# Fused tap mixing and two feed-forward layers: low parts made in other places and other forms

## What is computed

```python
def _attn_ref(x, weight):                       # x (2, 4096, 192), weight (8, 7)
    w = softmax(weight, axis=-1)
    x_pad = np.concatenate([zeros(B, 6, D), x], axis=1)
    x_unf = x_pad[:, idx, :].reshape(B, S, K, H, group)      # idx = s + k
    return np.einsum('hk,bskhg->bshg', w, x_unf).reshape(B, S, D)

def _moe_ref(x, w_gate, w_val, w_out):          # (8192, 192) -> 1536 -> 192
    g = x @ w_gate
    return (g * (1.0 / (1.0 + np.exp(-g))) * (x @ w_val)) @ w_out

def _moe2_ref(x, w_in, w_out):                  # (8192, 192) -> 2048 -> 192
    h = x @ w_in
    g = np.where(h > 0.0, h, np.exp(np.minimum(h, 0.0)) - 1.0)
    return g @ w_out
```

## Time and profile before

| | us |
|---|---|
| median of 3 runs | 1207.09 (1205.83 to 1207.34) |
| the profiled execution | 1206.76 |
| its span, first to last instruction | 1205.0 |
| PE busy (matmul) | 1199.5, 100% of the span |
| DVE busy | 775.5, 64% |
| POOL busy | 717.9, 60% |
| ACT busy | 664.2, 55% |
| granted TensorE clock | 1.000 in the whole span |

### The profile page before, as it was taken

The page is one execution under the profiler, slowest core; times in us unless marked ns, Lnnn a source line. Parts: engine busy times, 40 slices in busy tenths (PEclk is TensorE's granted clock), DMA queues, the critical chain, the costliest instruction groups (busy, mean ns, idle before and its releaser), DMA issues.

```text
span 1205.0 us, 31390 instructions
## 1 busy us (share of the span) xinstructions
PE 1199.5 (100%) x11798; PEld 1032.4 (86%) x11798; DVE 775.5 (64%) x1178; ACT 664.2 (55%) x1114; POOL 717.9 (60%) x528
## 2 busy tenths in 40 slices
PE   9999999999999999999999999999999999999999
PEld 7988888888888888889888898888988889888898
DVE  6787575675656756567665666656666476675665
ACT  6456555465554645546455464655546556465565
POOL 6787656574654746547465474654746557465565
PEclk9999999999999999999999999999999999999999
DMA  7412012120111211012110121100212002120110
GB/s 179 109 51 44 12 27 41 32 44 11 32 31 30 44 30 23 21 30 44 30 27 17 30 44 30 35 17 22 44 30 41 11 22 44 30 44 9 30 34 15
DMA packets 103955, 43.37 MB, mean 36 GB/s; under 512 B 75888, under 2 KB 93936, under 8 KB 103920
## 3 DMA queue, kind: packets, MB, share of 16 engines
q1 hardware_dynamic: 103104, 42.29, 15.7%
q10 hardware_dynamic: 816, 0.59, 0.2%
HBM read 16.12 MB, written 6.29 MB: 19 GB/s over the span
## 4 chain that ended last, share of the span: by engine, by line
PE 97%; POOL 1%; DVE 1%; issue 1%; ACT 0%; ACTq 0%; DVEq 0%
PE up L860 55%; PE down L860 42%; POOL hid_lo L441 1%; DVE mixed L830 0%; DVE act L771 0%; PE down L1063 0%; POOL up_w_lo L326 0%; DVE hidden L787 0%; ACT L617 0%; ACT hid_hi L608 0%; POOL y_main L445 0%; POOL halves L445 0%; DVE mixed L827 0%; DVE taps_head L813 0%; ACT act L593 0%
## 5 line engine op out<-in xcount | busy, mean ns | idle before, releaser
L441 POOL TENSOR_TENSOR hid_lo<-hidden,hid_hi 128x512 fp32r<-128x512 f32 x447 | 623.7, 1405 | 473.2 <-ACT hid_hi L574 304.8
L860 PE MATMUL down<-out_w,hid_hi 64*128 64x384 f32 x2040 | 300.4, 355 | 0.0
L734 DVE TENSOR_TENSOR hidden<-act,up 128x512 f32<-128x512 f32 x191 | 130.8, 685 | 249.1 <-ACT act L557 249.1
L860 PE MATMUL down<-out_w,hid_lo 64*128 64x192 f32 x2040 | 260.8, 251 | 0.3 <-POOL hid_lo L441 0.3
L771 DVE TENSOR_SCALAR act<-up 128x512 f32<-128x512 f32 x256 | 164.8, 685 | 112.0 <-PE up L860 112.0
L860 PE MATMUL up<-in_b_hi,up_w_hi 64*128 64x512 f32 x1128 | 224.1, 393 | 0.0
L860 PE MATMUL up<-in_b_hi,up_w_lo 64*128 64x512 f32 x1128 | 223.7, 393 | 0.0
L860 PE MATMUL up<-in_b_lo,up_w_hi 64*128 64x512 f32 x1128 | 223.6, 393 | 0.0
L574 ACT ACTIVATE hid_hi<-hidden 128x512 fp32r<-128x512 f32 x192 | 121.5, 633 | 177.9 <-DVE hidden L734 160.5
L608 ACT ACTIVATE hid_hi<-hidden 128x512 fp32r<-128x512 f32 x256 | 156.9, 628 | 96.5 <-DVE hidden L787 79.4
L593 ACT ACTIVATE act<-act 128x512 f32<-128x512 f32 x256 | 156.1, 631 | 94.8 <-DVE act L771 94.8
(11 more groups left out here) (96 smaller groups left out, 1085.9 us busy)
## 6 DMA issues: line engine op xcount, KB each, us to landing
x_raw<-x_dram SPq DMA_DIRECT2D x136, 64.0 KB, 2.2
out_dram<-stage SPq DMA_DIRECT2D x15, 384.0 KB, 2.7
in_b_hi<-in_b_hi SPq DMA_DIRECT2D x32, 128.0 KB, 2.3
in_b_lo<-in_b_lo SPq DMA_DIRECT2D x32, 128.0 KB, 2.3
swapped<-halves SPq DMA_DIRECT2D x32, 128.0 KB, 2.3
in_a_hi<-in_a_hi SPq DMA_DIRECT2D x30, 128.0 KB, 2.3
in_a_lo<-in_a_lo SPq DMA_DIRECT2D x30, 128.0 KB, 2.3
stage<-w_out_dram SPq DMA_DIRECT2D x7, 384.0 KB, 3.9
```

The source lines that it names most:

```text
L441: return pool.tensor_tensor(hid_lo[:, slot, :], hidden[:, s, :], hid_hi[:, slot, :].bitcast(F32), ALU.subtract)
L734: v.tensor_tensor(hidden[:, f % 2, :], act[:, f % 2, :], val_bank(f, n)[:, :], ALU.mult)\
L860: return nc.tensor.matmul(dst, lhsT, rhs, start=start, stop=stop, skip_group_check=True)
```

## The change

- `zero`, a tile of one column, is added, set by a further memset at the start (ZEROED 6 in place of 5).
- The first taps (steps 1 and 2 of `mix`) and `input_lo` become scalar-tensor-tensor instructions: x times tap plus `zero` (broadcast over 512 columns), and full times 1.0 less the high part.
- Chunk 1's taps, mixed beside chunk 0, follow a table `MIX_AT0`: 2, 3, 2, 2, 1, 3, 2, 1 steps behind products 2 to 9, and the two transposes stand behind product 2 in place of product 1. For all later chunks `MIX_AT` gives the old order.
- Piece 5 of the weights is split behind block 2 of chunk 0 in place of block 1, on ACT and POOL.
- The low part of piece 16 goes from DVE to POOL, at the same j; one semaphore `piece_lo` counts all low parts.

```diff
-        ZEROED = 5
+        ZEROED = 6
+        MIX_AT0 = {2: range(0, 2), 3: range(2, 5), 4: range(5, 7), 5: range(7, 9), 6: range(9, 10),
+                   7: range(10, 13), 8: range(13, 15), 9: range(15, 16)}
+        MIX_AT = {2: range(0, 1), **{3 + k: range(2 * k + 1, 2 * k + 3) for k in range(TAPS)},
+                  3 + TAPS: range(MIX - 1, MIX)}
...
-                              ("out", 1, "pool"), ("up", 6, "pool"), ("out", 2, "dve"), ("out", 3, "pool")):
+                         ("out", 1), ("up", 6), ("out", 2), ("out", 3)):
...
-        BESIDE0 = {1: 5, 3: 6, 5: 7, 7: 8, 8: 9}
+        BESIDE0 = {2: 5, 3: 6, 5: 7, 7: 8, 8: 9}
...
             eng.wait_ge(piece_hi, upto)
-            for who, made in (("dve", piece_lo_dve), ("pool", piece_lo_pool)):
-                if lo_count(upto, who):
-                    eng.wait_ge(made, lo_count(upto, who))
+            eng.wait_ge(piece_lo, lo_count(upto))
...
-                        v.tensor_scalar(mixed[:, part, :], src, tap, None, ALU.mult)\
-                            .then_inc(mix_step, 1)
+                        v.scalar_tensor_tensor(mixed[:, part, :], src, tap, zero[:, 0:1].broadcast_to([P, T]),
+                                               ALU.mult, ALU.add).then_inc(mix_step, 1)
...
-                v.tensor_tensor(dst["lo"][:, slot, :], full, dst["hi"][:, slot, :].bitcast(F32), ALU.subtract)\
-                    .then_inc(lo_sem, 1)
+                v.scalar_tensor_tensor(dst["lo"][:, slot, :], full, 1.0, dst["hi"][:, slot, :].bitcast(F32),
+                                       ALU.mult, ALU.subtract).then_inc(lo_sem, 1)
...
-                    if f == 1 and is_int(n, 0):
+                    if f == 2 and is_int(n, 0):
                         transpose_x(1, 0)
                         transpose_x(1, 1)
...
-                    at = 2 if is_int(n, 0) else 3
-                    if f == at - 1:
-                        mix(n + 1, 0)
-                    if at <= f < at + TAPS:
-                        mix(n + 1, 2 * (f - at) + 1)
-                        mix(n + 1, 2 * (f - at) + 2)
-                    if f == at + TAPS:
-                        mix(n + 1, MIX - 1)
+                    for step in (MIX_AT0 if is_int(n, 0) else MIX_AT).get(f, ()):
+                        mix(n + 1, step)
...
-            elu_phase(1, beside(BESIDE_ELU1, lambda i: make_lo(v, i, "dve")))
+            elu_phase(1)
```

More of the change, by code:

```diff
@@ L123, in mix_ffn_ffn @@
         y_tail = sb("y_tail", [P, T])
+        zero = sb("zero", [P, 1])
         result = stage[:, 0, :].rearrange("p (b d) -> p b d", d=D)
@@ L249, in up1_piece, with up2_piece @@
             hi, lo = up1_w["hi"][:, :, c0:c1], up1_w["lo"][:, :, c0:c1]
-            pieces.append((loads, [(hi, s)], [(lo, s, hi)], who))
-        def up2_piece(j0, j1, who):
+            pieces.append((loads, [(hi, s)], [(lo, s, hi)]))
+        def up2_piece(j0, j1):
             s = stage[:, len(pieces) % STAGES, 0:PARTS * (j1 - j0) * P].rearrange("p (g c) -> p g c", g=PARTS)
@@ L256, in up2_piece, with out_piece @@
             hi, lo = up2_w["hi"][:, :, j0 * P:j1 * P], up2_w["lo"][:, :, j0 * P:j1 * P]
-            pieces.append((loads, [(hi, s)], [(lo, s, hi)], who))
-        def out_piece(rows, dst, q, order, who):
+            pieces.append((loads, [(hi, s)], [(lo, s, hi)]))
+        def out_piece(rows, dst, q, order):
             s = stage[:, len(pieces) % STAGES, 0:OT * D].rearrange("p (f d) -> p f d", d=D)
@@ L263, in out_piece @@
             los = [(t[:, :, to:to + n], s[:, :, of:of + n], t[:, :, of:of + n]) for to, of, n in order]
-            pieces.append((loads, [(t[:, :, 0:D], s)], los, who))
+            pieces.append((loads, [(t[:, :, 0:D], s)], los))
         def out1_piece(q):
-            out_piece(wo1_rows, out1_w, q, [(D, P, TAIL), (D + TAIL, 0, P)], "pool")
+            out_piece(wo1_rows, out1_w, q, [(D, P, TAIL), (D + TAIL, 0, P)])
         UP1_AT, OUT1_AT = {}, {}
-        for what, at, who in (("up", 0, "pool"), ("up", 1, "pool"), ("up", 2, "pool"), ("out", 0, "pool"),
-                              ("up", 3, "pool"), ("up", 4, "pool"), ("out", 1, "pool"), ("up", 5, "pool"),
-                              ("up", 6, "pool"), ("out", 2, "pool")):
+        for what, at in (("up", 0), ("up", 1), ("up", 2), ("out", 0),
+                         ("up", 3), ("up", 4), ("out", 1), ("up", 5), ("up", 6), ("out", 2)):
             if what == "up":
-                up1_piece(at, who)
+                up1_piece(at)
                 UP1_AT[GROUPS[at][0] // P] = len(pieces)
@@ L281, in mix_ffn_ffn @@
         UP2_AT, OUT2_AT = {}, {}
[L282 to L283 removed]
+        for what, at in (("up", 0), ("up", 2), ("out", 0), ("up", 4),
+                         ("out", 1), ("up", 6), ("out", 2), ("out", 3)):
             if what == "up":
[L285 removed]
+                up2_piece(at, at + 2)
                 UP2_AT[at] = len(pieces)
             else:
[L288 removed]
+                out_piece(wo2_rows, out2_w, at, [(D, 0, D)])
                 OUT2_AT[at * OT] = len(pieces)
         AHEAD, READY = 6, 5
[L292 removed]
+        BESIDE0 = {2: 5, 3: 6, 5: 7, 7: 8, 8: 9}
         BESIDE1 = {0: 10, 1: 11, 9: 12, 10: 13, 11: 14}
@@ L299, in beside, with lo_count @@
             return lambda at: make(table[at]) if at in table else None
-        def lo_count(upto, who):
-            return sum(len(p[2]) for p in pieces[:upto] if p[3] == who)
+        def lo_count(upto):
+            return sum(len(p[2]) for p in pieces[:upto])
         def wait_weights(eng, upto):
             eng.wait_ge(piece_hi, upto)
-            for who, made in (("dve", piece_lo_dve), ("pool", piece_lo_pool)):
-                if lo_count(upto, who):
-                    eng.wait_ge(made, lo_count(upto, who))
+            eng.wait_ge(piece_lo, lo_count(upto))
         def stage_full(i):
@@ L319, in make_hi, with make_lo @@
                 nc.scalar.activation(dst, src, ACT.Copy).then_inc(piece_hi, 1)
-        def make_lo(eng, i, who):
-            if pieces[i][3] != who:
-                return
-            eng.wait_ge(piece_hi, i + 1)
+        def make_lo(pool, i):
+            pool.wait_ge(piece_hi, i + 1)
             for dst, src, hi in pieces[i][2]:
-                ins = eng.tensor_tensor(dst, src, hi.bitcast(F32), ALU.subtract)
-                ins.then_inc(piece_lo_dve if who == "dve" else piece_lo_pool, 1)
+                pool.tensor_tensor(dst, src, hi.bitcast(F32), ALU.subtract).then_inc(piece_lo, 1)
         def store_tokens(eng, m, blocks=slice(0, BLOCKS)):
@@ L490, in _ @@
             for i in range(READY):
[L491 to L492 removed]
+                make_lo(pool, i)
+            lo = lambda i: make_lo(pool, i)
             mix_phase(0, beside(BESIDE0, lo))
@@ L797, in _ @@
             v.memset(tap_pairs[:, :], 0.0).then_inc(zeroed, 1)
+            v.memset(zero[:, :], 0.0).then_inc(zeroed, 1)
             step = [0]
```

10 lines of the change are left out of this document (2 added, 8 removed).

## The result

The changed kernel takes **1208.96 us** in the median of 11 runs (1207.32 to 1209.72), the kernel before, run beside it, 1206.17 (11 runs, 1204.62 to 1207.46): a ratio of 1.002, interval 1.001 to 1.0029. It is slower by some 2.8 us, where the forecast was 0.8. The profiled execution took 1207.44, its span 1205.2, only 0.2 more than the span before. From that matmul on, the changed kernel is 1.4 us longer.

What follows compares the result with a forecast made beforehand. PE was taken as the bound, with no matmul removed. Chunk 0's +0.54 and piece 16's +0.28 gave +0.8 on the profiled 1206.76, 1207.6; the median's 0.33 above that execution made 1207.9, range 1206.0 to 1209.6.

Steps and rivals of the forecast that it cites:

- (c): Rival: the scalar-tensor-tensor form takes twice a tap's 0.74 us; +2.3 in chunk 0, 1209.4 in all; chance 0.05.
- (d): Rival: in chunk 0 one stall runs into the next, five blocks late by 0.3 to 0.5; +2, 1210; chance 0.09.
- `down1(0)` no longer waits: Block 3 of chunk 0: product 2 ends at 21.8, so PE's wait for it goes; minus 0.19 us.
- block 5: Chunk 0: product 3 comes just in time at 26.8 but PE finds its weights late; plus 0.08 us.
- block 6: Chunk 0: three taps ahead of product 4 delay PE's start from 30.21 to 30.48; plus 0.27 and 0.08 us.
- block 7: Chunk 0: product 5 was to end at 33.3, in time by 0.2 to 0.4; no loss for PE.
- block 10: Chunk 0: three taps ahead of product 8 take turns with POOL, product 8 at 43.75; plus 0.22 and 0.08 us.
- old losses of chunk 1: Second layer: both losses, 0.68 and 0.49, put down to piece 16 on DVE, would go; minus 1.17 us.
- wait for piece 16: Chunk 1's second layer: PE waits for POOL's piece 16 ahead of `down2_pair` of k = 8; plus 1.45, bounds 0.9 and 2.0.
- by the same steps product 5 ends at 33.3: Chunk 0: DVE and POOL taking turns as for product 4 would finish product 5 in time by 0.2 to 0.4 us.
- at a hand-over the one that has waited goes next: Timing rule for DVE's two-SBUF-input instructions against POOL's subtractions: whoever comes second ends 1.15 (POOL) or 0.55 (DVE) after the other.
- three signs of being wrong: A PE wait in the loop, piece 16 ending before 116, or taps with `zero` over 0.9 alone.

## Why the prediction was right in kind and too small

**The sum.** Forecast 1207.9 in a range of 1206.0 to 1209.6, measured 1208.96. The direction and the range are right, but the forecast of +0.8 is 2.0 short of the medians' difference. That the time still came within 1.1 is partly luck: the forecast started from a median of 3 runs, 1207.09, and the 11 beside the changed kernel gave 1206.17. The chances gave 0.90 to a difference under 2.4 us and 0.07 to a larger loss; the measured 2.8 is above that line, though its interval of 1.2 to 3.5 spans it. The upper part of the range was there for (c) and (d), which did not happen. Step by step, in what PE lost:

| term | forecast | traces of the changed kernel |
|---|---|---|
| `down1(0)` no longer waits | -0.19 | -0.26, with 0.07 at the pair behind |
| block 5 | +0.08 | +0.29 |
| block 6 | +0.35 | +0.29 |
| block 7 | 0 | +0.90 |
| block 10 | +0.30 | +0.44 |
| old losses of chunk 1 | -1.17 | -1.29, but in part of before's executions only |
| wait for piece 16 | +1.45 | +1.04; 1.48 or 1.49 in three relatives, where DVE gets in |

The last two rows are lengths of the second layer over the loop's 32.80; the forecast had missed 0.11 of the old losses, at the pair behind 122.32. The first five sum to +1.66, where the forecast had +0.54 and a bound of +1.5.

**The step that failed in chunk 0** is "by the same steps product 5 ends at 33.3", in time by 0.2 to 0.4. In the time scale of before (1.28 later) product 5 ended at 34.6. The rule beneath it, "at a hand-over the one that has waited goes next", does not hold for a tap issued 0.1 us ahead of the end of POOL's instruction, and piece 6 is two instructions in a row, so that missing one hand-over costs a whole further one. I had a lost hand-over in my bounds at half a microsecond. Here it cost the tap 1.24 (it ends at 31.04, and would have ended 0.55 behind POOL's 29.25), far more than my margin of 0.2 to 0.4. Moving piece 6 away removed exactly this loss. It is no draw: in all five traces with this order and piece 6 in its place, the tap is issued 0.08 ahead of the end and passed over. The trace of before had the same miss in a place I did not read, its first tap behind product 2:

```profile
22.25 3.60 DVE L686 TENSOR_SCALAR mixed<-x_t,taps 128x512 f32<-128x512 f32 x2
22.29 1.84 POOL L326 TENSOR_TENSOR up_w_lo<-stage,up_w_hi 128x768 fp32r<-128x768 f32 x1
```

POOL's instruction ahead of piece 5 ends at 22.33, 0.08 behind the tap's issue, and the tap still stands behind the whole piece and ends at 24.41.

**The step that failed in the second layer** is the same rule with the opposite sign, twice. `input_lo` did not get in ahead of the fold, though it had waited 0.8 us: the term of 1.45 came out as 1.04. The forecast had this case as 117.1 in its working, 0.5 ahead of its 117.6, and near its lower bound. And the minus of 1.17 took one trace for the kernel. Of before's three traces two lose it (34.1) and one does not (32.86), with DVE's instruction issued at the same place. Being passed over, twice in a row, costs 1.25 there. The head has two outcomes of its own, 12.65 and 13.93. Both together predict spans of about 1202.6, 1203.8 to 1204.1 and 1205.1. (The first of these, early head and no lost turn, was not traced.) Of 75 further executions of before, 8 lie at 1202.5 to 1202.9, 38 at 1203.7 to 1204.7 and 29 at 1205.0 to 1205.9: the three groups are there, blurred by the end of the program, which varies by up to 0.8. The profiled execution that the forecast started from was of the uppermost group, late head and lost turn.

That also closes most of the gap between 1.75, the difference of traces with like heads, and 2.8. The mean span of those 75 is about 1204.3, that of 21 executions of the changed kernel 1206.6, a difference of 2.3. The medians differ by more than the means, since that of before sits near the edge of two groups. Chunk 0 gives 1.7. In the changed kernel the second layer costs 33.85 where DVE stays out and about 34.3 where it gets in (traced with piece 6 moved, with the old forms and with piece 16 alone), so in no trace does it reach the 32.86 that one trace of before has. With 34.1 as a middle and before at 32.86 + 1.25 x 0.6, the share of lost turns that the three groups ask for when about two heads in three are late (9 of 14 traces), this gives 34.1 - 33.6 = 0.5, an estimate, and 2.2 in all. Had I read more than one execution of before, the 1.17 would have been 0.7.

None of the three signs of being wrong that the prediction named has appeared. They looked at the loop, at piece 16 and at the new taps alone, and none at chunk 0's hand-overs.

**The forms.** In the loop they cost nothing, as forecast: steps of PE unchanged to a hundredth over 13 chunks, first taps 0.74 alone (25.54 above) with the broadcast tile. By the Trainium skill's "Vector Engine (DVE) Microarchitecture Reference", section "Points that are easy to get wrong", they would have run at half the rate; the trace disagrees, 0.74 for this instruction. In chunk 0 they are worth 0.4 to 0.5 on PE (37.64 against 37.12 with the old order, 38.86 against 38.42 with the new one). Rival (c) is excluded. Rival (d), a stall that runs on, was right about the tight stretch and wrong about the cause: blocks 5 and 6 did not carry over into 7. With the old forms their losses are gone and block 7 still loses 0.85; with piece 6 moved they stay and block 7 loses nothing.

**What stays open.** Why DVE gets its turn in chunk 1's second layer in some executions and is passed over in others. Having waited 0.3, it was passed over twice in a row in two traces of the kernel before and let in in the third. Having waited 0.8, it was passed over twice in both traces of the changed kernel and in the one with chunk 0's old order, and let in with the old forms, with piece 6 moved and with piece 16 alone. Whether a gap on POOL would make it certain was not tried.

## What to carry to other kernels

Where DVE with two SBUF inputs and POOL share a stretch that PE waits on, price each meeting with one lost turn (here 1.2 us), above all where POOL has two instructions in a row, and don't trust an order that needs DVE to get in when it is issued less than 0.1 us ahead of POOL's end. Read two or three traces of the kernel before: a loss of 1.2 us in one may be a draw of that execution, and a change that removes it has only a part of it to gain. Compare stages by PE's starts, not spans, since a head that came 1.28 early hid nearly all of this loss.
